# All loads from one queue, six opened tiles and three moved roundings in a gated-scan ELU feed-forward kernel

## What is computed

```
sig = 1 / (1 + exp(-f_logit))
f = lower_bound + (1 - lower_bound) * sig          # per channel
h = 0
for t in range(6080):
    h = f[:, t] * h + (1 - f[:, t]) * x[:, t]
    y[:, t] = h

hid = y @ w_in                                     # 256 -> 2048
g = where(hid > 0, hid, exp(min(hid, 0)) - 1)      # ELU
out = g @ w_out                                    # 2048 -> 256
```

## Time and profile before

| | us |
|---|---|
| median of 3 runs | 1010.96 |
| lowest and highest | 1010.54, 1011.62 |
| the profiled execution, its own time | 1011.16 |
| its span, first to last instruction | 1009.3 |
| PE busy | 1003.2 (99% of the span) |
| ACT busy | 794.6 (79%) |
| DVE busy | 728.9 (72%) |
| POOL busy | 632.9 (63%) |

### The profile page before, as it was taken

One profiled execution on the slowest core, in us unless ns is written; L12 is line 12 of the kernel. 1 busy time (PEld: TensorE's weight loads), 2 busy tenths in 40 slices (PEclk: granted clock), 3 DMA queues, 4 the chain that ended last, 5 costly groups with the idle time before them and its releaser, 6 DMA issues.

```text
span 1009.3 us, 15356 instructions
## 1 busy us (share of the span) xinstructions
PE 1003.2 (99%) x4362; PEld 816.4 (81%) x4362; DVE 728.9 (72%) x913; ACT 794.6 (79%) x1427; POOL 632.9 (63%) x474
## 2 busy tenths in 40 slices
PE   8999999999999999999999999999999999999998
PEld 5788778888888888888888888888888888888997
DVE  6785886785787687688669669758867966875544
ACT  7997778877877777877787787787788778778775
POOL 2584897567557557656655755756675575566454
PEclk9999999999999999999999999999999999999999
DMA  7211102101201110210120120021021011000101
GB/s 271 63 32 43 54 1 74 53 1 52 73 0 32 41 51 0 73 52 0 55 70 0 42 60 24 6 66 52 0 62 62 0 42 60 12 0 5 40 1 37
DMA packets 23211, 41.88 MB, mean 41 GB/s; under 512 B 2704, under 2 KB 4240, under 8 KB 23184
## 3 DMA queue, kind: packets, MB, share of 16 engines
q1 hardware_dynamic: 22752, 41.04, 12.7%
q10 hardware_dynamic: 432, 0.53, 0.2%
HBM read 29.10 MB, written 12.45 MB: 41 GB/s over the span
## 4 chain that ended last, share of the span: by engine, by line
PE 97%; DVE 1%; issue 1%; DMA 1%; ACT 0%; ACTq 0%; DVEq 0%
PE acc L858 17%; PE acc L856 17%; PE acc L857 17%; PE h L828 14%; PE h L830 14%; PE h L832 13%; PE h L951 1%; PE h L952 1%; PE h L953 1%; DMA x<-value 1%; DVE x L599 0%; DVE x L591 0%; PE acc L952 0%; PE acc L953 0%; PE acc L951 0%
## 5 line engine op out<-in xcount | busy, mean ns | idle before, releaser
L314 POOL TENSOR_TENSOR g_lo<-e,g_hi 128x512 fp32r<-128x512 f32 (+1 forms) x384 | 517.3, 1356 | 370.7 <-ACT g_hi L452 370.4
L438 ACT ACTIVATE e<-h 128x512 f32<-128x512 f32 (+1 forms) x380 | 226.4, 596 | 163.6 <-PE h L832 128.3
L690 DVE SCALAR_TENSOR_TENSOR e<-e,h 128x512 f32<-128x512 f32 (+1 forms) x380 | 257.3, 677 | 80.0 <-ACT e L444 79.8
L858 PE MATMUL acc<-g_hi,w_out_lo 128*128 128x512 f32 (+1 forms) x768 | 301.9, 393 | 0.0
L856 PE MATMUL acc<-g_hi,w_out_hi 128*128 128x512 f32 (+1 forms) x768 | 301.0, 392 | 0.0
L857 PE MATMUL acc<-g_lo,w_out_hi 128*128 128x512 f32 (+1 forms) x768 | 299.7, 390 | 0.0
L452 ACT CAST g_hi<-e 128x512 fp32r<-128x512 f32 (+1 forms) x384 | 233.1, 607 | 22.3 <-DVE e L690 22.3
L444 ACT ACTIVATE e<-e 128x512 f32<-128x512 f32 (+1 forms) x384 | 242.1, 630 | 8.4
L828 PE MATMUL h<-a_hi,w_in_hi 128*128 128x512 f32 (+1 forms) x616 | 241.2, 392 | 0.3 <-DVE h L676 0.3
L830 PE MATMUL h<-a_lo,w_in_hi 128*128 128x512 f32 (+1 forms) x616 | 240.6, 391 | 0.0
L832 PE MATMUL h<-a_hi,w_in_lo 128*128 128x512 f32 (+1 forms) x616 | 238.8, 388 | 0.0
(11 more groups left out here) (64 smaller groups left out, 571.4 us busy)
## 6 DMA issues: line engine op xcount, KB each, us to landing
out<-out_sb SPq DMA_DIRECT2D x44, 256.0 KB, 2.1
gate<-forget_logit SPq DMA_DIRECT2D x43, 256.0 KB, 2.7
x<-value SPq DMA_DIRECT2D x43, 256.0 KB, 2.8
w_in_raw<-w_in SPq DMA_DIRECT2D x8, 256.0 KB, 6.4
w_out_raw<-w_out SPq DMA_DIRECT2D x8, 256.0 KB, 7.7
x<-value SPq DMA_DIRECT2D x4, 224.0 KB, 2.6
gate<-forget_logit SPq DMA_DIRECT2D x4, 224.0 KB, 2.5
out<-out_sb SPq DMA_DIRECT2D x4, 224.0 KB, 2.0
```

Source lines behind the costliest of these rows:

```text
L314: nc.gpsimd.tensor_tensor(g_lo[:, t % RING, 0:w], e[:, t % TILES, 0:w], g_hi[:, t % RING, 0:w].bitcast(F32), ALU.subtract).then_inc(g_lo_r ...
L438: nc.scalar.activation(e[:, i, 0:w], bank_of(j, t)[:, 0:w], ACT.Relu, scale=-1.0).then_inc(r_ready, 1)
L690: nc.vector.scalar_tensor_tensor(e[:, t % TILES, 0:w], e[:, t % TILES, 0:w], -1.0, bank_of(j, t)[:, 0:w], ALU.add, ALU.max).then_inc(g_rea ...
L858: done = nc.tensor.matmul(bank, lo, g_hi[:, t % RING, 0:w], start=False, stop=closes)
```

## The change

There are four parts. SP now begins all loads but that of the bound: gate and x of sequence 0, both halves, ahead of the weights; ACT's two loads are gone. `first_products` opens six tiles in place of four: tiles 4 and 5 used to be whole `first_product`s, and their high-by-high matmuls now stand in the two opening groups. For that, `round_plain(2)` on ACT moves ahead of `split_first(0, 1)`. The rounding of w_out for pairs 1, 2 and 3 moves from ACT to DVE, behind the same tiles 0, 2 and 5. And the matmuls on zeros are 20 in place of 18.

```
-WARM_UP = 18
+OPEN = 6
+WARM_UP = 20
...
-            load_gate(0, 0, 0)
-            load_x(0, 0, 0)
+            for i in range(HALVES):
+                load_gate(0, 0, i)
+                load_x(0, 0, i)
             load_w_in(0)
...
-                if t in (0, 2, 5, 7, 8, 10, 15):
-                    round_w_out({0: 1, 2: 2, 5: 3, 7: 4, 8: 5, 10: 6, 15: 7}[t])
+                if t in (7, 8, 10, 15):
+                    round_w_out({7: 4, 8: 5, 10: 6, 15: 7}[t])
...
-            act.dma_start(gate[:, 0, 1], forget_logit[0, :, 1, tokens(0)]).then_inc(gate_loaded[0][1], 16)
-            act.dma_start(x[:, 0, 1], value[0, :, 1, tokens(0)]).then_inc(x_loaded[0][1], 16)
             for i in range(HALVES):
                 tanh(0, 0, i)
                 open_gate(0, 0, i)
             round_plain(0)
             split_first(0, 0)
             round_plain(1)
+            round_plain(2)
             split_first(0, 1)
-            round_plain(2)
             round_w_out(0)
...
+            def round_w_out(p):
+                dve.wait_ge(w_out_loaded[p], 16)
+                nc.vector.tensor_copy(w_out_hi[:, p], w_out_raw[:, p]).then_inc(w_out_hi_ready[p], 1)
+
             def first_spare(t):
                 if t in (0, 1, 2, 3, 14):
                     w_plain_rest({0: 3, 1: 4, 2: 5, 3: 6, 14: 7}[t])
+                if t in (0, 2, 5):
+                    round_w_out({0: 1, 2: 2, 5: 3}[t])
...
-                    for unit in range(TILES):
+                    for unit in range(OPEN):
                         pe.wait_ge(w_plain_hi_ready, unit // 2 + 1)
...
-                for unit in range(TILES):
+                for unit in range(OPEN):
                     bank = first_bank(unit)
...
-                    done.then_inc(done_of[unit], 1)
+                    done.then_inc(done_of[unit % TILES], 1)
...
-            for t in range(TILES, TILES * PAIRS):
+            for t in range(OPEN, TILES * PAIRS):
                 first_product(t)
```

## The result

The changed kernel takes 1014.23 us, median of 10 runs (1013.73 to 1014.55), against 1011.45 (1010.54 to 1012.57) for the kernel before on the same chip. The ratio is 1.0028, with a 95% interval of 1.0019 to 1.0036: slower by 2.8 us, where a gain of 1.4 had been predicted. The profiled execution took 1014.55 us with a span of 1012.7. Its span is 3.4 longer than that of before, a little more than the medians differ.

The account below looks back on a forecast made before the run. TensorE was taken as the bound; 0.56 + 0.45 + 0.1 + 0.3 = 1.4 us off the profiled 1011.16 gave 1009.76, or 1009.5 against the median. The forecast's own range was 1009.1 to 1010.0, the full range 1009.0 to 1010.9.

Parts of the forecast that it names:

- What bounds it: Whole kernel: TensorE, busy 1003.2 of 1009.3 us, so only fewer matmuls or its idle time can save time.
- The sum: Whole kernel: gains at the start and tile 10 total 1.4 us; nothing after tile 10 adds or gives back.
- The loads: Start: x of half 1 lands at about 6.0, near the byte bound, making `weigh` of half 1 0.56 us earlier.
- Rival 1: Start: the loads come no earlier, leaving a gain of 0.75 us, time 1010.2; chance 0.15.
- Six opened tiles: Opening groups: two more matmuls fill TensorE's idle time, 0.45 us, plus 0.1 us for a hidden weight load.
- rival 2: Start: the third w_in load lands late and its rounding delays the second split to 10.15, time 1010.6; chance 0.10.
- The copies: Tiles 0 to 6: three roundings on DVE at 0.6 us each; a shorter stall at tile 10 gains 0.3 us.
- Rival 3: Tiles 0 to 10: copies collide with POOL at 1.56 us each, delaying tile 10, time 1011.5; chance 0.10.

Follow-up runs that it names:

- e8: Kernel before with the new loads, six opened tiles, and the w_out roundings of pairs 5, 6, 7 moved to VectorE instead of 1, 2, 3: 1013.1 us.
- e1: Kernel before with the new order of loads alone: 1011.07 us, ratio 0.9998.
- e2: Kernel before with six opened tiles, 20 matmuls on zeros and the earlier `round_plain(2)` alone: 1011.91 us, ratio 1.0006.
- e10: Kernel before with six opened tiles, old loads, and ScalarE's w_out roundings and their subtractions behind later tiles: 1010.51 us, ratio 0.9994.
- e12: Kernel before with only ScalarE's w_out roundings and their subtractions put behind later tiles: 1010.67 us, ratio 0.9995.

## Why the prediction was wrong

**What bounds it** was right: TensorE's idle time decides. "All of this change is therefore settled in the first 30 us" was the step that cost most. It was read from a profile in which TensorE has one short wait behind 30 us (0.31 us at 129.80, overlooked, and the same in both kernels), and it says nothing on a kernel whose programs have other lengths. The sum put what follows tile 10 at nothing for the same reason. Of 3.4 us, 1.6 came behind 932 us. The time of 1014.23 lies beyond the 1013.0 to which the prediction gave 0.02, and none of its rivals reaches it.

**The loads** were to bring 0.56 us and brought none. SP began them at 1.65 (gate of half 1) and 2.12 (x of half 1), and the DMA view of the changed kernel, windows at the start, has

```profile
x<-value SPq DMA_DIRECT2D x1, 256.0 KB, 3.0
...
gate<-forget_logit SPq DMA_DIRECT2D x1, 256.0 KB, 4.7
x<-value SPq DMA_DIRECT2D x1, 256.0 KB, 4.9
```

x of half 1 landed at 2.12 + 4.9 = 7.0, where 6.0 was forecast, and the gate ahead of it at 1.65 + 4.7 = 6.35, where before had it at 5.4. ScalarE's timeline shows the gate now as what the start waits for:

```profile
6.40 0.63 ACT L396 ACTIVATE gate<-gate 128x512 f32<-128x512 f32 x1 [1.36 <-DMA gate<-forget_logit]
```

`weigh` of half 1 began at 8.04 in place of 7.69, not at 7.13. That execution was a late one, but no other reached the forecast either. In the twelve kernels with the new order the gate landed at 5.67 to 7.02 and x at 6.47 to 7.67; in the six with the old one the gate landed at 5.09 to 5.51 and x at 7.30 to 7.97. So x did come earlier, by less than forecast, and the gate later. With the old order split 2 stands 2.07 us behind the landing of x, with the new one 3.71 behind that of the gate (3.98 in e8), which makes 9.37 to 10.04 the one way and 9.38 to 10.72 the other. The 0.56 us would have needed the gate at about 5.5.

The failed step is the landing taken near the bound by bytes. The gate was third of one queue, and by 6.38 us the engines had moved 213 GB/s x 6.38 us = 1.36 MB, which is 5.2 transfers:

```profile
0.00:6.38 6.38, 5.06 (x14) 1.87 (x15) 1.46 (x5) 2.73 (x3) 0.73 (x5) 1.00 0.71 213
```

When the second transfer had landed, at 4.14, it was 169 GB/s x 4.14 us = 0.70 MB, 2.7 transfers. All of them but the small one of the bound came from one queue, so sharing between queues can't be the reason: within the one queue bytes of later transfers moved before the third was complete. Why is open. Rival 1, loads no earlier, was the case, and its number (a late gate "near 6.2") was close. In e1 this costs nothing: the gate landed at 6.03 and the second split stands at 9.74 as before.

**Six opened tiles** did what was said. The two matmuls of 0.23 us took the place of idle time: from split 2 to `first_product(6)` it is 7.60 us in place of 8.05, the forecast 0.45. With the second split at 10.09 in place of 9.74, `first_product(6)` began at 17.69 against 17.79: 0.10 gained. The working had that tile 0 is finished behind a group of six, but counted it against a start 0.56 earlier. Without that start, the elu of tile 0 comes 0.8 us later (14.66 against 13.85: 0.35 from the later split, 0.45 from the two matmuls ahead of it), while TensorE comes to tile 10 earlier. That alone is e2: tile 10 waits 1.05, and the opening loses 0.44 from split 2 to mark 1. What TensorE wins at the start it waits for at the first bank that it needs back.

**The third weights** didn't hold the split (rival 2): ScalarE did `round_plain(2)` without a wait.

**The copies** were sized well, 0.42, 0.41 and 0.49 us for a forecast of 0.6. Missing was the instruction behind each. The prediction looked at the copy alone and asked whether POOL was busy when the copy starts; the two-source subtraction behind it used to fit in front of POOL's operation, and 0.46 us later on one side with 0.53 earlier on the other put it behind. The step freed on ScalarE, booked as pure gain, was half of the collision. Two such subtractions cost 1.06 and 1.0 us, and the `weigh` ahead of the elu of tile 7 1.1. The elu of tile 6 was forecast for 27.1 and came at 29.54.

**Rival 3** has the right outcome by a wrong way. It gave the elu of tile 6 at 29.1, tile 10 at 29.8 and 1011.5; measured were 29.54 and 30.29. Its copies of 1.56 us were not seen; the collision was in the subtraction. It was given 0.10, and it had no wait at tile 11 and none at the exit. Its elu of tile 1 doesn't follow from its own terms either: 13.85 - 0.2 for the elu of tile 0, then 0.6 + 0.6 + 1.56 + 0.6 is 17.0, where it has 16.7.

**The sum.** At tile 10 TensorE is 1.11 us late: 0.10 gained, 1.21 lost in the wait (1.38 for 0.17). At tile 11 the step from the matmul before is 33.66 - 32.91 = 0.75 in place of 0.23, so 0.5 more. That is 1.6 of the 1.75 at mark 1, the other 0.1 isn't placed, and the exit's 1.6 makes 3.4, as the spans differ. The medians differ by 2.8. What the change costs apart from the start of that one execution, 1.40 in block 0 and 1.6 at the exit, is 3.0.

## What to carry to other kernels

When an instruction is put ahead of others on an engine, look at each instruction that it pushes back, and at what the other engine on the same port will have begun by then; what the move frees elsewhere can bring that begin forward, and the moved instruction's own length can be the smallest part. Before the difference of two profiles at a mark is put down to a change, measure from the last landing that the start waits for: here that took 0.7 us of scatter down to 0.03. When a start is sped up, follow it to the first buffer that must come back, and see whether the engine that frees it has been sped up as well. And when a change alters how many instructions an engine has ahead of a straight-line piece behind a loop, look for idle time marked "issue" there, and try one or two instructions more before judging the change.

## What was not expected of the hardware

ScalarE stands 1.9 us at a fixed instruction of block 11, 4.4 us after the end of its loop, when its program ahead is 5 instructions shorter than before's, and not with 4, 3, 2 or 0 fewer; it costs TensorE 1.6 us. Before has a shorter gap of that kind, harmless where it falls, three instructions ahead in the list:

```profile
928.98 0.57 ACT L423 CAST a_hi<-x 128x448 fp32r<-128x448 f32 x1 [0.85 <-issue]
```

All four kernels with 0 fewer have it (before, e2, e10, e12; 0.81 to 1.16 us; e10, with the longest, has an exit 0.2 us longer), and in the ten kernels where it is 2 to 4 fewer ahead of block 11 the timeline marks no such gap. One transfer of 256 KB, third of a queue, landed when the bytes of 5.2 had moved. And a subtraction that starts 0.11 us behind POOL's takes 1.74 us in place of 0.69.
